# Early loads of a linear-attention and feed-forward kernel: which landing each one waits for

## What is computed

```python
for t in range(S):                      # per batch and head
    cur = outer(u * k[t], v[t])
    y[t] = r[t] @ (state + cur)
    state = w[t][:, None] * state + outer(k[t], v[t])
x = y as (3072, 384)
x = (x @ w_a) * (x @ w_b) @ w_out       # width 1536
h = x @ w_in2                           # width 2048
out = (max(h, 0) + alpha * min(h, 0)) @ w_out2
```

## Time and profile before

| | us |
|---|---|
| median of 3 runs | 1031.2 |
| lowest, highest | 1030.21, 1034.61 |
| the profiled execution, its own time | 1032.22 |
| its span, first to last instruction | 1030.4 |
| TensorE busy in it | 1004.4 (97%) |
| VectorE, ScalarE, GpSimd busy | 560.0, 288.7, 24.3 |
| mean granted TensorE clock | 0.993 |

### The profile page before, as it was taken

How to read it: one execution, slowest core, us unless ns; L and a number is a source line. 1 busy time by engine, 2 the same in 40 slices (tenths; PEclk the granted TensorE clock), 3 DMA queues, 4 the chain that set the end, 5 groups by cost and what they waited for, 6 DMA issues and landing times.

```text
span 1030.4 us, 29090 instructions
## 1 busy us (share of the span) xinstructions
PE 1004.4 (97%) x12448; PEld 980.0 (95%) x12448; DVE 560.0 (54%) x1170; ACT 288.7 (28%) x604; POOL 24.3 (2%) x24
## 2 busy tenths in 40 slices
PE   5699999999999999999999999999999999999998
PEld 5599999999999999999999999999999999999998
DVE  7477665654655656556542446645554545545454
ACT  3424414224133242241222433222222222222211
POOL 4400000000000000000000000000000000000000
PEclk9889999999999999999999999999999999999999
DMA  5464231301312113011020223010101010101000
GB/s 139 115 164 127 56 102 30 90 25 33 86 52 64 30 52 91 3 55 34 26 59 1 85 85 98 26 47 1 47 1 47 1 46 0 46 0 46 4 21 24
DMA packets 42167, 53.01 MB, mean 51 GB/s; under 512 B 5184, under 2 KB 42048, under 8 KB 42048
## 3 DMA queue, kind: packets, MB, share of 16 engines
q1 hardware_dynamic: 40624, 51.04, 17.4%
q10 hardware_dynamic: 1424, 0.23, 0.1%
HBM read 39.46 MB, written 9.44 MB: 47 GB/s over the span
## 4 chain that ended last, share of the span: by engine, by line
PE 96%; DMA 1%; DVE 1%; ACT 1%; issue 1%; ACTq 0%; DVEq 0%; SPq 0%
PE products L166 18%; PE products L167 16%; PE products L168 16%; PE acc L166 11%; PE acc L168 11%; PE acc L167 11%; PE products L695 5%; PE products L710 1%; PE products L739 1%; PE products L755 1%; PE products L672 1%; PE products L724 1%; DMA k_in<-in_k_dram 1%; DMA stage<-in_w_out_dram 0%; DMA x_parts<-f_y 0%
## 5 line engine op out<-in xcount | busy, mean ns | idle before, releaser
L166 PE MATMUL products<-x_parts,weights_hi 128*128 128x384 f32 x576 | 201.9, 351 | 3.6 <-DMA x_parts<-f_y 1.1
L167 PE MATMUL products<-x_parts,weights_hi 128*128 128x384 f32 x576 | 195.3, 339 | 0.0
L168 PE MATMUL products<-x_parts,weights_lo 128*128 128x384 f32 x576 | 194.9, 338 | 0.0
L1238 DVE TENSOR_SCALAR leaky_low<-products,leaky_al 128x384 f32<-128x384 f32 x128 | 79.0, 618 | 169.5 <-PE products L168 169.4
L1098 DVE TENSOR_TENSOR g_sb<-a_g,products 128x384 f32<-128x384 f32 x96 | 53.2, 554 | 197.9 <-issue 133.3
L1185 ACT ACTIVATE leaky_g_hi<-leaky_g_sb 128x384 fp32r<-128x384 f32 x128 | 67.3, 525 | 295.0 <-DVE leaky_g_sb L1243 295.0
L513 ACT ACTIVATE g_hi<-g_sb 128x384 fp32r<-128x384 f32 x96 | 50.4, 524 | 255.7 <-DVE g_sb L1098 255.7
L166 PEld LDWEIGHTS products<-x_parts,weights_hi 128*128 128x128 f32 x576 | 108.9, 189 | 8.5 <-issue 4.6
L168 PEld LDWEIGHTS products<-x_parts,weights_lo 128*128 128x128 f32 x576 | 109.1, 189 | 0.0
L167 PEld LDWEIGHTS products<-x_parts,weights_hi 128*128 128x128 f32 x576 | 109.1, 189 | 0.0
L166 PE MATMUL acc<-g_hi,weights_hi 128*128 128x384 f32 x288 | 97.5, 339 | 0.0
(11 more groups left out here) (85 smaller groups left out, 1758.1 us busy)
## 6 DMA issues: line engine op xcount, KB each, us to landing
k_in<-in_k_dram SPq DMA_DIRECT2D x16, 336.0 KB, 4.2
r_in<-in_r_dram SPq DMA_DIRECT2D x16, 336.0 KB, 5.2
stage<-in_w_out_dram SPq DMA_DIRECT2D x14, 384.0 KB, 3.3
w_v<-in_v_dram SPq DMA_DIRECT2D x16, 288.0 KB, 3.6
y_dram<-x_in SPq DMA_DIRECT2D x8, 576.0 KB, 3.2
x_in<-y_dram SPq DMA_DIRECT2D x8, 576.0 KB, 4.5
out_dram<-leaky_out_sb SPq DMA_DIRECT2D x7, 576.0 KB, 3.3
stage<-in_w_dram SPq DMA_DIRECT2D x10, 336.0 KB, 3.8
```

What stands on the lines that cost most here:

```text
L166: pe.matmul(out, w_hi, x_hi, start=first, stop=False)
L167: pe.matmul(out, w_hi, x_lo, start=False, stop=False)
L168: return pe.matmul(out, w_lo, x_hi, start=False, stop=last)
L1238: dve.tensor_scalar(self.low[f % 2][:, :], h, 0.0, self.al[:, f:f + 1], ALU.min, ALU.mult).then_inc(self.low_ready, 1)
```

## The change

Only SyncE's program changes. In step 2, the first v load waits for piece 1 to have landed and the second for piece 2, where each waited behind itself for its own landing. The first r load waits for the first v, the second r for the second v; nothing behind it waits for an r load. At the start, pieces 0 and 1 are issued one after the other, and piece 2 waits for piece 0.

```diff
--- before.py
+++ after.py
@@ -408,14 +408,14 @@
                     n, phase = divmod(step, PHASES)
                     if phase == 2:
                         for j in range(2):
+                            if n == 0:
+                                sp.wait_ge(shared.staged[1 + j], shared.staged_by[1 + j])
                             load_v(n, j)
-                            if n == 0:
-                                sp.wait_ge(v_loaded[j], 16)
                         if n + 1 < DUOS:
                             for j in range(2):
+                                if n == 0:
+                                    sp.wait_ge(v_loaded[j], 16)
                                 load_r(n + 1, j)
-                                if n == 0:
-                                    sp.wait_ge(r_loaded[2 + j], 16)
                         if STAGED_FROM <= n + 1 < DUOS:
                             load_w(n + 1, 0)
                             load_w(n + 1, 1)
@@ -439,8 +439,9 @@
                 load_w(0, 1)
                 sp.wait_ge(w_loaded[1], 16)
                 for piece in range(STAGES):
+                    if piece == 2:
+                        sp.wait_ge(shared.staged[0], shared.staged_by[0])
                     shared.load_piece(sp, piece)
-                    sp.wait_ge(shared.staged[piece], shared.staged_by[piece])
                 for step in range(BEFORE_TILES):
                     attend(step)
                     for piece in early_at(LOAD_AT, step):
```

## The result

| | before | changed |
|---|---|---|
| median, us | 1031.35 (12 runs) | 1024.46 (12 runs) |
| lowest to highest | 1030.18 to 1034.61 | 1023.0 to 1028.78 |
| profiled execution, its own time and span | 1032.22, 1030.4 | 1024.34, 1022.5 |
| mean granted clock in it | 0.993 | 1.000 |

The ratio is 0.9938, with a 95% interval of 0.9924 to 0.9952: 6.9 us faster, inside the predicted range and on the predicted side, 2.9 us above the predicted 1021.6.

A forecast was written before the change was run, and what follows sets the result against it. The first attention step was held by the late k load, after which TensorE's own work would bind. The first up product ending 9.85 us earlier, less 0.2, gives 9.65 off 1031.2: 1021.6 us, range 1019.6 to 1026.

The forecast's parts named there:

- The bound: First attention step: its end hangs on the late k_in load, then x_parts' move and 18 matmuls at half clock.
- Pieces, v and r: SyncE's early loads: piece 1 lands about 18.6, r is issued at 24.6 to 28.7, queue free by 25 to 29.
- Nobody gains: Pieces 0 to 2 landing earlier help no engine, since GpSimd splits them only from 29.42 on.
- k: Both k loads wait only for the turned keys, go out at 28.9 and 30.4, the second landing by 36.2.
- ScalarE and the leaf matmuls: Last output copies start at 40.4, 6.5 us earlier; the next step's leaf matmuls follow at once, 40.4 to 43.2.
- The moves and the first up product: Moves of x_parts land by 46.0; the up product runs 43.2 to 47.3 at full clock, 0.8 idle.
- w: Next step's w load lands by 49.1, just before VectorE reaches it at 49.2, so no wait.
- The 0.2 for the accumulator's copy: Next up product waits for ScalarE's accumulator copy, formerly covered by slow matmuls: 0.2 us off the gain.
- The sum: First up product ends 9.85 us earlier, some 2.8 of it clock; less 0.2, a gain of 9.65.
- The first rival: TensorE's clock falls anyway around the first up product, 43 to 49: gain only 7.1 to 8.0; chance 0.18.
- The held k: Second k load really waits for TensorE's last output matmuls, going at 38.4: gain 2.1, 1029 us; chance 0.05.
- the slower rival: Clock falls at 43 and stays low through the second attention step, to about 77: 1036 us; chance 0.03.

The follow-up runs named there:

- e2: Kernel before with only the new start of pieces 0 to 2; v and r loads still waited for singly: 1027.96 us, ratio 0.9966.
- e5: Changed kernel with pieces, v and r loads all held until the last level of stream 0: 1034.15 us.
- e4: The kernel before, unedited, profiled a second time: 1031.37 us.
- e0: The changed kernel, unedited, measured and profiled again: 1022.92 us, ratio 0.9913.
- e3: Changed kernel with the three starting pieces waited for singly again, v and r loads as changed: 1024.8 us, ratio 0.9929.
- e11: Changed kernel with no early load waiting for a landing, same kernel as e10, run again with more rounds: 1023.77 us, ratio 0.9925.
- e1: Changed kernel with the second r load also waiting for the first r load to land: 1024.48 us, ratio 0.9936.
- e7: Changed kernel with the r loads waiting for no landing: 1022.91 us, ratio 0.9921.
- e10: Changed kernel with no early load (pieces 0 to 2, v, r) waiting for a landing: 1022.47 us, ratio 0.9922.
- e9: Changed kernel with r loads waiting for no landing, and pieces 3 and 4 held until both k loads have landed: 1025.86 us, ratio 0.9949.

## Why the prediction was right, and what it missed

*The bound.* Right. The wait for k was what the first step's end hung on; taking it away moved the output copies, and 7.2 us of shift at 54.57 (the level matmuls that started at 61.80 before) became 7.8 at 68.24 (76.02 before), as small idle times closed, and 7.9 in the span.

*Pieces, v and r.* Right to within 1 us: v at 19.55 (18.6), r at 24.32 (24.6). "Nobody gains" of the pieces is right for the whole change; alone they give 3.2 (e2).

*k.* The rule was right, the number wrong: k went when the keys were turned, but these came at 31.5 and 32.8, not 28.9 and 30.4. This is the step that failed, "k goes out at 28.9 and 30.4 whatever the queue does before". It took TensorE's times from a profile in which no instruction block was late. Up to 45 us such stops sum to 1.0 to 3.2 us in every other profiled execution but e5, 1.5 of them even in the kernel before, where the late k covered them (e4). The landings themselves were on the safe side: the second k took 4.3 for the assumed 5.8.

*ScalarE and the leaf matmuls.* Right in order and slack: 0.17 us of wait for k, and the leaf matmuls follow the outputs without a gap but for 0.30 of stop.

*The moves and the first up product.* 47.3 predicted, 49.4 measured: 2.1 late, the 2.3 of the stop among it. *w* held, with more room than the 0.1 us that was forecast (landed at 49.5 and 51.0, first used at 51.31 and 52.25): VectorE doesn't wait. The 0.2 for the accumulator's copy was right in kind (a gap from 49.43 to 49.66).

*The sum.* 9.65 predicted; the profiled executions differ by 7.9, so 1.75 are missing: the 2.1 us of lateness above, less what the closed idle times gave back. The medians differ by 6.9. That last 1.0 is mostly a matter of which executions were profiled: the kernel before took 1032.22 in its own, 0.9 above its median of 1031.35, the changed kernel 1024.34, 0.1 below its own.

*The first rival.* The mean clock fell a little in a part of the executions. Of the changed kernel's twelve, seven have a mean clock of 1.00 and take 1023.7 on average, five have 0.996 to 0.998 and take 1027.0; without the five the median is 1023.75, so they put 0.7 us on it. In e0's four it is 1.00 each time. The rival had a chance of 0.18 and a cost of 1.7 to 2.5; a lower clock came in 5 of 12, at 3.3 between the groups. A mean of 0.997 over 1025 us is about 3.1 us of clock (an estimate), so the difference can be almost all clock. That it is the fall between 43 and 49 that the rival describes isn't shown: both profiles of the changed kernel have a mean of 1.00. The profiles that have such a fall are of e3 and e11 (last section). The held k and the slower rival didn't come about.

## What to carry to other kernels

When a change takes away the wait that bounds a stage, go through what that wait had covered, stops that show as "issue" among them: one profile without them doesn't say that they aren't there, and when they come it is at the same instructions. The second profile of the kernel before (e4) has 1.5 us of them, where the first has none; a second profile can show what the first does not. And once a load is bound to the work that frees its buffer, as k is here, a finer or looser pacing of what goes before it was no longer seen in the time (e1, e7, e10, e11).

## What was not expected of the hardware

A stretch of small matmuls, 126 recorded ones to a block of instructions and a block every 4 to 6 us, can be short of instructions: stops of 0.4 us or more in 12 of the 14 profiled executions, up to 2.3 for one. Loads were on the way at some time before all of these, but as said they are not shown to be the reason.

The clock doesn't follow from the length of one idle time. In e9 TensorE was idle for 3.24 us before 45.86, and the clock stayed at 1.00 (last fence of e9, and in every window after it to 60). In e11 it was idle for 2.26 before 44.98, and the granted clock was 1.00 from 45 to 46, 0.57 in the next microsecond and then 0.50; in e3 it was idle for 2.77, and the clock fell at once. The first four rows are of e11, the last two of e3:

```profile
44.98 0.41 PE L166 MATMUL products<-x_parts,weights_hi 128*128 128x384 f32 x1 [2.26 <-DMA x_parts<-f_y]
...
45.00:46.00 1.00, 1.00 (x6) 1.00 (x7) 0.00 (x0) 0.00 (x0) 0.94 (x1) 1.00 0.73 140
46.00:47.00 1.00, 1.00 (x5) 1.00 (x4) 0.00 (x0) 0.00 (x0) 0.89 (x1) 0.57 1.05 361
49.00:50.00 1.00, 1.00 (x5) 0.87 (x4) 0.00 (x0) 0.49 (x1) 0.00 (x0) 0.72 1.15 290
...
47.07 0.53 PE L166 MATMUL products<-x_parts,weights_hi 128*128 128x384 f32 x1 [2.77 <-DMA x_parts<-f_y]
...
47.00:48.00 1.00, 0.93 (x3) 0.96 (x4) 0.00 (x0) 0.03 (x1) 0.89 (x1) 0.61 0.65 111
```

The dense matmuls of e11 thus ran at 1.2 GHz from some point after 46 until past 49, those of e3 from 47 until past 50. Summed over the windows of 1 us, the missing clock is 1.7 us of work in each (an estimate), at the lower end of the rival's 1.7 to 2.5. The Trainium skill, TensorE: Matmul & The Clock Gate, section A second HAM failure mode: psum-queue depth-cycling, tells of a clock that goes back and forth when TensorE is idle for short times between groups of matmuls. Neither profile shows that: each has one fall and one rise, behind one idle time that is longer than any the changed kernel's two profiles have here (1.13 and 1.36 us). What happened in the 5 of 12 executions with a lower mean clock, no profile shows.
